# Attention's V loaded over 128 partitions: key spans in pairs, pooling rows in groups of 128 and 16

## What is computed

```python
def _attn_ref(q, k, v):
    B, H, S, D = q.shape
    factor = 4
    ...
    q_d = q.reshape(B, H, Sd, factor, D).mean(axis=3)      # k_d, v_d alike
    out_d = sm_attn(q_d, k_d, v_d)                         # 144 pooled positions
    out_up = np.repeat(out_d, factor, axis=2)
    mask = np.abs(pos[:, None] - pos[None, :]) < factor    # local: 3 keys each side
    ...
    out_local = np.matmul(attn, v)
    return (out_up + out_local).astype(np.float32)

def reference(**kwargs):
    attn_out = _attn_ref(**attn_kwargs)
    x = attn_out.transpose(0, 2, 1, 3).reshape(B * S, H * D)
    x = _moe_ref(x=x, **moe_kwargs)          # x @ w_in, h * tanh(softplus(h)), @ w_out
    return _moe2_ref(x=x, **moe2_kwargs)     # x @ w_in, h * softmax(h), layer norm, @ w_out
```

## Time and profile before

| | us |
|---|---|
| median of three executions | 711.88 |
| the profiled execution's own time | 715.35 |
| its span, first to last instruction | 713.5 |
| PE busy in the span | 685.6 (96%) |
| DVE busy | 369.0 (52%) |
| ACT busy | 263.2 (37%) |
| POOL busy | 184.3 (26%) |
| last local value matmuls start | 105.70 |

### The profile page before, as it was taken

One profiled execution on the slowest core, in us unless ns is written; L12 is line 12 of the kernel. 1 busy time (PEld: TensorE's weight loads), 2 busy tenths in 40 slices (PEclk: granted clock), 3 DMA queues, 4 the chain that ended last, 5 costly groups with the idle time before them and its releaser, 6 DMA issues.

```text
span 713.5 us, 12623 instructions
## 1 busy us (share of the span) xinstructions
PE 685.6 (96%) x5098; PEld 634.0 (89%) x5098; DVE 369.0 (52%) x686; ACT 263.2 (37%) x583; POOL 184.3 (26%) x228
## 2 busy tenths in 40 slices
PE   6879879999999999999999999999989999999998
PEld 5768679999999999999999999999868888888886
DVE  7988957543233222322232223474796667666671
ACT  5868755332111211121121111135653544444441
POOL 5988920000000000000000000484535434354100
PEclk9988989999999999999999999999999999999999
DMA  8997983000000000000000030002200000000001
GB/s 232 253 204 211 253 304 119 0 1 1 1 1 0 1 1 1 1 1 0 1 1 1 1 118 1 1 1 60 60 16 16 29 31 15 16 30 29 31 16 44
DMA packets 24185, 37.51 MB, mean 53 GB/s; under 512 B 2624, under 2 KB 12864, under 8 KB 24000
## 3 DMA queue, kind: packets, MB, share of 16 engines
q1 hardware_dynamic: 24128, 36.71, 17.5%
HBM read 31.99 MB, written 4.72 MB: 51 GB/s over the span
## 4 chain that ended last, share of the span: by engine, by line
PE 83%; POOL 9%; issue 4%; DVE 3%; DMA 1%; ACT 1%; SPq 0%; POOLq 0%; DVEq 0%
PE psum L668 28%; PE psum L682 28%; PE psum L772 12%; PE psum L749 11%; POOL half_v L495 2%; PE psum L758 2%; POOL half_qk L482 2%; POOL prob L503 1%; POOL vd L496 1%; POOL qd L485 1%; POOL ylo L546 1%; DMA kT<-kT_dram 1%; DVE so L1276 1%; POOL kd L485 0%; PE psum L654 0%
## 5 line engine op out<-in xcount | busy, mean ns | idle before, releaser
L1173 DVE CAST ghi<-g_sb 128x384 fp32r<-128x384 f32 x96 | 39.7, 414 | 246.1 <-PE psum L682 189.2
L887 ACT ACTIVATE g_sb<-psum 128x384 f32<-128x384 f32 x96 | 47.2, 492 | 295.9 <-PE psum L668 292.3
L668 PE MATMUL psum<-xhi,whi 128*128 128x384 f32 x384 | 130.6, 340 | 1.7 <-issue 1.1
L668 PE MATMUL psum<-xlo,whi 128*128 128x384 f32 x384 | 130.1, 339 | 0.0
L668 PE MATMUL psum<-xhi,wlo 128*128 128x384 f32 x384 | 130.0, 338 | 0.0
L682 PE MATMUL psum<-ghi,wlo 128*128 128x384 f32 x384 | 129.0, 336 | 0.0
L682 PE MATMUL psum<-ghi,whi 128*128 128x384 f32 x384 | 129.0, 336 | 0.0
L682 PE MATMUL psum<-glo,whi 128*128 128x384 f32 x384 | 129.0, 336 | 0.0
L518 POOL TENSOR_TENSOR t<-raw 128x1024 f32<-128x1024 f32 x1 | 2.6, 2640 | 356.5 <-PE psum L682 356.5
L668 PEld LDWEIGHTS psum<-xhi,whi 128*128 128x128 f32 x384 | 73.0, 190 | 2.5 <-issue 1.7
L668 PEld LDWEIGHTS psum<-xlo,whi 128*128 128x128 f32 x384 | 73.1, 190 | 0.0
(11 more groups left out here) (121 smaller groups left out, 1065.4 us busy)
## 6 DMA issues: line engine op xcount, KB each, us to landing
wraw<-w_dram SPq DMA_DIRECT2D x12, 512.0 KB, 5.1
qT<-qT_dram SPq DMA_DIRECT2D x16, 288.0 KB, 4.5
kT<-kT_dram SPq DMA_DIRECT2D x16, 288.0 KB, 5.9
v<-v_dram SPq DMA_DIRECT2D x16, 288.0 KB
out_dram<-ob SPq DMA_DIRECT2D x18, 256.0 KB, 2.0
vw<-v_dram SPq DMA_DIRECT2D x32, 128.0 KB, 3.9
wraw<-w_dram SPq DMA_DIRECT2D x16, 256.0 KB, 5.7
raw<-w_dram SPq DMA_DIRECT2D x1, 2048.0 KB, 7.4
```

Source lines behind the costliest of these rows:

```text
L668: ins = nc.tensor.matmul(bank, a[:, w], b[:, kdx, :], start=(kdx == 0 and n == 0), stop=(kdx == KD - 1 and n == 2))
L887: nc.scalar.activation(g_sb[:, f % HR, :], psum[:, HB1 + f % HB, 0:N1], ACT.Mish).then_inc(g_ok, 1)
L1173: nc.vector.tensor_copy(ghi[:, f % GR, :], g_sb[:, f % HR, :]).then_inc(ghi_ok, 1)
```

## The change

The window loads become five DMAs a unit, one for each slot. Each fills 128 partitions by 512 B: its source runs over 2 spans, each of 64 keys. For pooling, v is loaded as 128 rows of four keys (2 KB) and 16 rows of four keys, in two DMAs, into the tile `v4`; pooled keys 0 to 127 are group 0 and 128 to 143 are group 1. The second group's other 112 partitions are cleared once by DVE, since POOL adds over all 128 partitions, and so is a part of PSUM that ACT's copy reads. TensorE takes neighbouring columns when it turns the pooled probabilities, 128 and 16, and contracts over 128 and 16 keys.

```diff
-PQ = POOLED // 2
+PT = POOLED - P
...
-        v8 = sb("v8", [PQ, 2, 8 * P])
+        v4 = sb("v4", [P, 2, 2, POOLF * P])
...
-        vd = sb("vd", [PQ, 2, 2, P])
+        vd = sb("vd", [P, 2, 2, P])
...
-        half_v = sb("half_v", [PQ, 4 * P])
+        half_v = sb("half_v", [P, 2, 2 * P])
...
-        pprobT = sb("pprobT", [PQ, 2, NPB, 2, PB])
+        pprobT = sb("pprobT", [P, 2, NPB, 2, PB])
...
-        VW_DMAS = 4
+        VW_DMAS = NP
...
-                for jp, i0, n in ((0, 0, 1), (0, 1, NP - 1), (1, 0, NP - 1), (1, NP - 1, 1)):
-                    src = bass.AP(v_u.tensor, v_u.offset + window(i0, jp) * P,
-                                  [[P, KW], [PSTEP * P, n], [1, P]])
-                    sp.dma_start(vw[jp * KW:(jp + 1) * KW, par, i0:i0 + n, :], src).then_inc(ld_vw[par], 16)
+
+                for i in range(NP):
+                    src = bass.AP(v_u.tensor, v_u.offset + window(i, 0) * P,
+                                  [[(window(i, 1) - window(i, 0)) * P, 2], [P, KW], [1, P]])
+                    sp.dma_start(vw[:, par, i, :], src).then_inc(ld_vw[par], 16)
...
-                    sp.dma_start(v8[:, u % 2, :], v_d[u].rearrange("(p t) c -> p (t c)", t=8))\
-                      .then_inc(ld_v8[u % 2], 16)
+                    if u == 0:
+                        sp.wait_ge(rest_ok, 2)
+                    sp.dma_start(v4[:, u % 2, 0, :], v_d[u][0:POOLF * P].rearrange("(p t) c -> p (t c)", t=POOLF))\
+                      .then_inc(ld_v4[u % 2], 16)
+                    sp.dma_start(v4[0:PT, u % 2, 1, :], v_d[u][POOLF * P:SEQ].rearrange("(p t) c -> p (t c)", t=POOLF))\
+                      .then_inc(ld_v4[u % 2], 16)
...
-                pool.wait_ge(ld_v8[par], 16 * (u // 2 + 1))
+                pool.wait_ge(ld_v4[par], 32 * (u // 2 + 1))
...
-                t2 = half_v[:, :].rearrange("p (g c) -> p g c", g=2)
-                src = v8[:, par, :].rearrange("p (g c) -> p g c", g=2)
-                own(nc.gpsimd.tensor_tensor(t2, src[:, :, 0:2 * P], src[:, :, 2 * P:4 * P], ALU.add))
-                nc.gpsimd.tensor_tensor(vd[:, par, :, :], t2[:, :, 0:P], t2[:, :, P:2 * P], ALU.add)\
+                src = v4[:, par]
+                own(nc.gpsimd.tensor_tensor(half_v[:], src[:, :, 0:2 * P], src[:, :, 2 * P:4 * P], ALU.add))
+                nc.gpsimd.tensor_tensor(vd[:, par, :, :], half_v[:, :, 0:P], half_v[:, :, P:2 * P], ALU.add)\
...
-                for g in range(2):
+                for g, n in enumerate((P, PT)):
                     for b in range(NPB):
-                        src = pprob[0:PR, par, b, :].rearrange("p (i two) -> p two i", two=2)[:, g, :]
                         at = g * TP1 + b * PS
-                        ins = nc.tensor.transpose(turned[0:PQ, at:at + PR], src, ident[0:PR, 0:PR])
+                        ins = nc.tensor.transpose(turned[0:n, at:at + PR], pprob[0:PR, par, b, g * P:g * P + n],
+                                                  ident[0:PR, 0:PR])
...
-                    for g in range(2):
-                        ins = nc.tensor.matmul(turned[rows, OD0:OD0 + POOLED], vd[:, par, g, rows],
-                                               pprobT[:, g, :, h, :], start=(g == 0), stop=(g == 1))
+                    for g, n in enumerate((P, PT)):
+                        ins = nc.tensor.matmul(turned[rows, OD0:OD0 + POOLED], vd[0:n, par, g, rows],
+                                               pprobT[0:n, g, :, h, :], start=(g == 0), stop=(g == 1))
...
+            pe.wait_ge(rest_ok, 1)
...
+            nc.vector.memset(psum[:, PTB + 2, P:512], 0.0).then_inc(rest_ok, 1)
+            nc.vector.memset(v4[:, :, 1, :], 0.0).then_inc(rest_ok, 1)
             nc.vector.tensor_copy(identb[:], ident[:]).then_inc(identb_ok, 1)
```

More of the change, by code:

```diff
@@ L233, in program @@
         zero_ok = sem("zero_ok")
+        rest_ok = sem("rest_ok")
         ident_ok = sem("ident_ok")
@@ L242, in program @@
         ld_vw = [sem(f"ld_vw{i}") for i in range(2)]
-        ld_v8 = [sem(f"ld_v8_{i}") for i in range(2)]
+        ld_v4 = [sem(f"ld_v4_{i}") for i in range(2)]
         ld_wi = [sem(f"ld_wi{i}") for i in range(KD)]
@@ L849, in copy_pooled @@
                 wait(act, p_valued, u)
-                first = turned[0:PQ, 0:PB]
+                first = turned[:, 0:PB]
                 queries = bass.AP(first.tensor, first.offset, [first.ap[0], [TP1, 2], [HD, 2 * NPB], [1, PB]])
```

## The result

The changed kernel takes 778.76 us (median of six, 777.26 to 779.38), the kernel before 712.19: 1.091 times as long (95% interval 1.088 to 1.095). The forecast was 810, in a range of 764 to 848. The profiled executions took 777.26 and 715.35 us, 61.9 us apart; the medians are 66.6 apart, since the profiled execution before was 3.2 us over its median and the one after 1.5 under. All of the 61.9 lies in attention: the last local value matmuls end at 168.2 us for 106.5, and from there to the end of the span it is 607.3 us for 607.0.

What follows compares the result with a forecast made beforehand. POOL bounded attention before; window loads on two DMA engines would bound it after. Attention's +95.5 us and 2.6 us for the clock gave +98 on 715.35, 813.5, or 810 us against the median; range 764 to 848.

Steps and rivals of the forecast that it cites:

- Rivals A: Window loads use all 16 engines, so nothing slows: 713 us; chance 0.08.
- B: Window loads on 16 engines, but SP's slow window issues become the bound: 730 us; chance 0.03.
- C: Window loads on 16 engines and landing earlier, a small gain: 706 us (704 to 709); chance 0.04.
- Point 1: Window loads: 320 packets a unit on each of two engines at 30 ns, 9.6 us a unit against 5.1.
- point 6: Kernel start: DVE's clearing of PSUM and v4 delays it and PE's first scores by 1.0 us.
- point 4: End of attention: summed loads on the two engines put the last local value at 202.0 us, plus 95.5 us.
- Point 2: Other loads on the two engines: q and k 1.5, pooled v 0.8 us a unit; period 11.9 us.
- Point 3: Window queue in attention: never runs dry, compute of 5.1 us a unit fits under it, packets add without gaps.
- Point 5: After attention: PE starts the rest at the lower clock, adding 2.6 us.
- Point 7: POOL, PE and ACT work in attention: zero added cost, still zero if the forecast on the engines is wrong.
- Point 8: SP's issues: five window issues 3.1 us, 4.9 us a unit in all, hidden under 11.9.
- What would show it: Profile signs: 2080 small packets, window landing over 10 us, DMA share halved, chain naming vw, attention ending near 202 us.

Runs made afterwards that it cites:

- e4: The changed kernel with each window load reading four spans of 32 rows (not the right rows): 725.49 us, ratio 1.018.
- e5: The changed kernel with each window load reading eight spans of 16 rows (not the right rows): 712.07 us, ratio 1.000.
- e6: The changed kernel with each window load reading 127 neighbouring rows, and a sixth DMA filling the last partition: 897.23 us (one execution).
- e3: The changed kernel with each window load reading one run of 128 neighbouring rows instead of two spans of 64: 712.21 us, ratio 1.000.
- e8: The kernel before, with v laid out a second time by windows on the host and one window DMA a unit: 709.74 us, ratio 0.996.
- e9: The kernel of e8 with the change's pooling (groups of 128 and 16 keys): 713.22 us, ratio 0.999.
- e11: The kernel of e9 with pooled values looping over groups outside and heads inside: 710.39 us, ratio 0.996.
- e10: The kernel of e1 with v for pooling in two DMAs, of 64 and 8 partitions: 788.61 us, ratio 1.107.
- e1: The kernel before with the window loads alone changed, v for pooling still in 72 partitions: 786.87 us, ratio 1.106.
- e12: The kernel of e1 with v for pooling in two DMAs of 72 partitions with 2 KB rows: 782.95 us, ratio 1.095.

## Why the prediction was right, and where not

- **The mechanism: right.** Two engines by the count of completion packets (2080), and the same arithmetic held for outermost counts of 4, 8, 127 and 128 (e4, e5, e6, e3). The period is 9.74 us, where 11.9 was forecast. Rivals A, B and C needed 16 engines and are out. That the source's count binds, and not only the destination's, was inferred before; e3 to e5, with the same destination, show it.
- **Point 1, the price of a packet: too high, and it is nearly the whole miss.** 30 ns was taken, 23.2 measured (e4 against the change; e6 gives 23.7). 16 x 320 x 6.8 ns = 35 us; 202.0 us was forecast for the end of attention, 168.2 came. With 23.2 ns, and without the late start of point 6, the sum of point 4 gives 166 us, so that 2 us stay unexplained. The row behind the 34 ns gives busy time per packet while 16 engines run at once. A share can pass 1, as the front of this document says and the earlier trace rows shows, so busy times overlap, and busy time divided by packets is more than an engine needs. The changed kernel shows it on two engines: from 70.5 to 72.5 us, 173 packets at a share of 0.144 are 26.6 ns of busy time each, while two engines had only 23.1 ns for each. The lower bound, bytes at the rate of the weight loads (21 ns), was the nearer one; I weighed the two the wrong way.
- **Point 2: right.** 2.3 us forecast for q, k and pooled v, and 9.74 us less 320 x 23.2 ns leaves 2.3.
- **Point 3: right.** SP's issues stand back to back, and of its waits for a semaphore in attention, 23 us in all before, one of 3.2 us is left.
- **Point 5, the clock after attention: wrong by its 2.6 us.** What follows attention took 0.3 us more than before. I had forgotten that the hidden pieces, which run under the last wait, come before the rest: TensorE is busy with them all of 158.6 to 163.8 us, at a granted clock of 0.79 on average, and from 163.8 us on it is 1.00 in the stage table above.
- **Point 6, the start: 0 for 1.0 us,** at the lower bound.
- **Point 7, TensorE: wrong, but hidden.** "Zero" for the pooled values was 1.62 us for 0.72 a unit, since the weight loads alternate between 128 and 16 rows. With two engines as the bound no cost of it can be seen. Without them it fills TensorE: from 34.37 us of 40 in e8 to 38.65 in e9. Had the forecast on the engines failed, "still zero" would have held by a narrow margin only: e9 against e11 is 2.8 us.
- **Point 8: right that SP's 4.9 us are hidden,** but it took 3.1 us for the five window issues, and they lasted 6.8, 1.36 each. This is hidden as well, since the two engines are busy meanwhile.
- **What would show it:** past the first unit the chain does not name vw but "issue", and the time to landing isn't printed for vw. In no trace here is one printed for a DMA on fewer than 16 engines.

## What to carry to other kernels

Look at the outermost count of both sides of each DMA: in every run here it decided how many of the 16 engines worked. A source that begins with 2 cost 66 us and 127 rows cost 185, where filling 128 partitions saved nothing. Count the completion packets of a profile. A load without a time to landing is a hint, but no proof: in e5 and e10 v has none either, on 16 engines. A mean over 16 engines hides two full ones, and a price for a loaded engine is taken from bytes over time, or from two runs that differ in one load, not from packets' busy time.

## What was not expected of the hardware

- TensorE's weight loads stop for 0.2 us at each change between contractions over 128 and over 16 rows (three times a unit in e9, once in e11); between two groups of 72 rows they don't.
- DMAs on few engines, one behind the other, hold up the issuing queue: 0.47 us an issue of 128 rows of 512 B on 16 engines (e3), 0.75 to 0.80 on four (e4), 1.36 on two, and 2.4 for 127 rows on one (e6).
- One engine moves about 22 GB/s in rows of 512 B, whether one, two or four engines are the full ones (23.2 ns a row between four and two, 23.7 between two and one).
- With rows of 4 KB of pooled v among the two engines' short ones the kernel took 3.9 us more than with rows of 2 KB, at the same bytes (e1, e12).
